# Moving the computation of a branch flag from VectorE to GpSimd, in the first microseconds of a fused attention and MLP kernel

## The reference

```python
scores = scale * np.matmul(q, k.transpose(0, 1, 3, 2))
is_sink = pos[None, :] < int(n_sink)
rel = pos[:, None] - pos[None, :]
in_window = (rel >= 0) & (rel < int(window))
scores = np.where(is_sink | in_window, scores, -1e9)
a = softmax(scores); x = np.matmul(a, v)          # -> 1536 tokens of 512
h = x @ w_in; g = h * tanh(softplus(h)); x = g @ w_out          # first network, 2048 wide
for e in range(4):                                              # second, 4 experts of 1024
    out += p[:, e:e+1] * (relu(x @ w1[e]) @ w2[e])              # p: normalised domain_probs
```

## Time and profile before

| | us |
|---|---|
| median of 3 runs | 852.88 |
| lowest and highest of the runs | 852.72, 852.91 |
| the profiled execution | 852.87 |
| its span in the trace | 851.0 |
| TensorE busy in the span | 842.8 |
| VectorE, ScalarE, GpSimd busy | 605.4, 401.6, 172.1 |

### The profile page before, as it was taken

The page is one execution under the profiler, slowest core; times in us unless marked ns, Lnnn a source line. Parts: engine busy times, 40 slices in busy tenths (PEclk is TensorE's granted clock), DMA queues, the critical chain, the costliest instruction groups (busy, mean ns, idle before and its releaser), DMA issues.

```text
span 851.0 us, 13888 instructions
## 1 busy us (share of the span) xinstructions
PE 842.8 (99%) x4518; PEld 729.6 (86%) x4518; DVE 605.4 (71%) x1170; ACT 401.6 (47%) x739; POOL 172.1 (20%) x259
## 2 busy tenths in 40 slices
PE   7999999999999999999999999999999999999998
PEld 5777888888888888898999899889989998999897
DVE  7888799898888989876566565565565555656655
ACT  6999754448754549754324314314414413422410
POOL 6778200001100112222012112102202202202100
PEclk9999999999999999999999999999999999999999
DMA  7555730004830006825045135225225315403304
GB/s 257 143 162 154 159 100 1 1 0 97 194 106 0 0 0 127 162 59 115 19 104 117 28 89 117 43 74 117 56 61 117 68 49 117 92 25 68 69 0 151
DMA packets 25622, 72.70 MB, mean 85 GB/s; under 512 B 4336, under 2 KB 6512, under 8 KB 25584
## 3 DMA queue, kind: packets, MB, share of 16 engines
q0 software_dynamic: 10720, 33.82, 22.1%
q1 hardware_dynamic: 14576, 38.04, 13.1%
q10 hardware_dynamic: 288, 0.39, 0.1%
HBM read 35.28 MB, written 3.15 MB: 45 GB/s over the span
## 4 chain that ended last, share of the span: by engine, by line
PE 99%; DMA 0%; POOL 0%; DVE 0%; ACT 0%; issue 0%; SPq 0%; DVEq 0%
PE banks L944 31%; PE banks L870 28%; PE banks L839 15%; PE banks L636 15%; PE banks L651 3%; PE banks L732 3%; PE banks L702 3%; PE banks L738 1%; DMA pool<-kT 0%; POOL pool L480 0%; PE banks L705 0%; PE banks L957 0%; ACT pool L1067 0%; DVE pool L1863 0%; DVE pool L1486 0%
## 5 line engine op out<-in xcount | busy, mean ns | idle before, releaser
L1789 DVE SCALAR_TENSOR_TENSOR pool<-banks,p_norm,pool 128x512 f32<-128x512 f32 x179 | 132.8, 748 | 66.1 <-PE banks L944 64.3
L944 PE MATMUL banks<-w_hi,g_lo 128*128 128x512 f32 x382 | 149.9, 392 | 0.0
L944 PE MATMUL banks<-w_lo,g_hi 128*128 128x512 f32 x382 | 149.7, 392 | 0.0
L944 PE MATMUL banks<-w_hi,g_hi 128*128 128x512 f32 x382 | 148.7, 389 | 0.0
L1291 ACT ACTIVATE g_hi<-pool 128x384 fp32r<-128x384 f32 x96 | 50.5, 526 | 190.7 <-DVE pool L1769 139.1
L870 PE MATMUL banks<-x_hi,w_lo 128*128 128x384 f32 x256 | 86.0, 336 | 0.0
L870 PE MATMUL banks<-x_hi,w_hi 128*128 128x384 f32 x256 | 85.9, 335 | 0.0
L870 PE MATMUL banks<-x_lo,w_hi 128*128 128x384 f32 x256 | 85.7, 335 | 0.0
L944 PEld LDWEIGHTS banks<-w_hi,g_lo 128*128 128x128 f32 x382 | 71.7, 188 | 15.0
L944 PEld LDWEIGHTS banks<-w_hi,g_hi 128*128 128x128 f32 x382 | 71.7, 188 | 13.8 <-issue 0.2
L944 PEld LDWEIGHTS banks<-w_lo,g_hi 128*128 128x128 f32 x382 | 71.7, 188 | 13.8
(11 more groups left out here) (151 smaller groups left out, 1776.3 us busy)
## 6 DMA issues: line engine op xcount, KB each, us to landing
w_raw<-weights SPq DMA_DIRECT2D x48, 512.0 KB, 4.4
w_lo<-w_raw POOLq DMA_DIRECT2D x48, 512.0 KB, 5.5
w_lo<-w_sum POOLq DMA_DIRECT2D x15, 384.0 KB, 4.0
pool<-v SPq DMA_DIRECT2D x8, 384.0 KB, 3.5
out<-pool SPq DMA_DIRECT2D x11, 256.0 KB, 2.0
pool<-kT SPq DMA_DIRECT2D x7, 400.0 KB, 5.0
pool<-qT SPq DMA_DIRECT2D x7, 384.0 KB, 4.1
w_lo<-pool POOLq DMA_DIRECT2D x2, 384.0 KB, 4.9
```

What stands on the lines that cost most here:

```text
L944: mm = pe.matmul(banks[:, bank, :], g[:, s, f * SUP + at:f * SUP + at + P], w_cols(w, p2 * SLOT + DOWN_AT[f], DM), start=(f == 0 and n == ...
L1789: dve.scalar_tensor_tensor(out=to, in0=d_bank, scalar=share, in1=to, op0=ALU.mult, op1=ALU.add)\
```

## The change

The five small instructions that make `flag` leave VectorE and are done by GpSimd, behind its identity matrix and ahead of its wide masks, with a new semaphore `ok_made` between the dependent ones. They are written a little differently (one of them does the comparison of the second limit and the product at once). VectorE goes from `lim` straight to its masks. VectorE's read of the flag moves from behind the masking of unit 3 to between unit 1 and unit 2; its branch stays where it was. The other three engines' code is not touched.

```diff
+LIMIT_STEPS = 4
...
+            pl.wait_ge(setup, LIMIT_STEPS)
+            pl.tensor_scalar(ok[:, 0:1], lim[:, 0:1], 0.0, float(SINKS), ALU.max, ALU.min).then_inc(ok_made, 1)
+            pl.tensor_scalar(ok[:, 1:2], lim[:, 1:2], 1.0, float(P), ALU.max, ALU.min).then_inc(ok_made, 1)
+            pl.wait_ge(ok_made, 2)
+            pl.tensor_scalar(ok[:, 2:3], ok[:, 0:1], lim[:, 0:1], None, ALU.is_equal).then_inc(ok_made, 1)
+            pl.wait_ge(ok_made, 3)
+            pl.tensor_scalar(ok[:, 3:4], ok[:, 1:2], lim[:, 1:2], ok[:, 2:3], ALU.is_equal, ALU.mult).then_inc(ok_made, 1)
+            pl.wait_ge(ok_made, 4)
+            pl.tensor_copy(flag[:, :], ok[:, 3:4]).then_inc(flag_ready, 1)
...
-            dve.tensor_scalar(ok[:, 0:1], lim[:, 0:1], 0.0, float(SINKS), ALU.max, ALU.min).then_inc(setup, 1)
-            dve.tensor_scalar(ok[:, 1:2], lim[:, 1:2], 1.0, float(P), ALU.max, ALU.min).then_inc(setup, 1)
+            assert steps[0] == LIMIT_STEPS
             dve.wait_ge(iota_done, 3)
             mask_off(even + P, pos[:, :], sink_limit)
-            dve.wait_ge(setup, steps[0] + 2)
-            dve.tensor_tensor(ok[:, 2:4], ok[:, 0:2], lim[:, :], ALU.is_equal).then_inc(setup, 1)
             mask_off(MASK_AT[0], rel[:, P:], window_limit)
-            dve.wait_ge(setup, steps[0] + 3)
-            dve.tensor_tensor(ok[:, 0:1], ok[:, 2:3], ok[:, 3:4], ALU.mult).then_inc(setup, 1)
             mask_off(MASK_AT[1], rel[:, :], window_limit)
-            steps[0] += 4
-            dve.wait_ge(setup, steps[0])
-            dve.tensor_copy(flag[:, :], ok[:, 0:1]).then_inc(flag_ready, 1)
...
             dve.wait_ge(mask_ready, 5)
-            for u in range(4):
+            for u in range(2):
+                mask_unit(0, u)
+            dve.wait_ge(flag_ready, 1)
+            small = dve.value_load(flag[0:1, 0:1])
+            for u in range(2, 4):
                 mask_unit(0, u)
...
-            dve.wait_ge(flag_ready, 1)
-            small = dve.value_load(flag[0:1, 0:1])
             dve.br_cmp(small, 1, on_true="dve_window", on_false="dve_general", comp_op="IS_EQ")
```

More of the change, by code:

```diff
@@ L300, in build @@
         full_masked = sem("full_masked")
+        ok_made = sem("ok_made")
         qk_in = [sem(f"qk_in{b}") for b in range(B)]
```

## The result

| | us |
|---|---|
| changed kernel, median of 22 runs | 854.03 (853.91 to 854.70) |
| kernel before, median of 22 runs beside it | 852.87 (852.72 to 852.99) |
| ratio | 1.0015, interval 1.0008 to 1.0021 |
| profiled execution, span | 853.91, 852.1 |

The changed kernel is 1.16 us slower. That is inside the 0.2% that the prediction took for what a measurement can tell from no change, and 854.03 lies inside its range of 852.8 to 854.4. But it is nearly twice the 0.65 us of the forecast, it is just outside the "0.3 to 1.1 us slower" to which the prediction gave 0.70, and with 22 runs each the two sets do not overlap. So there is something to explain: half a microsecond.

The account below looks back on a forecast made before the run. The prediction took TensorE, busy 842.8 of 851.0 us, as the bound, movable only through its start at 11.25 us. Flag 0.82 us later less 0.17 slack, +0.65 on 852.87, gave 853.5 us, range 852.8 to 854.4.

Parts of the forecast that it names:

- 0.3 to 1.1 us slower: The forecast case: TensorE's scores of unit 4 wait behind the late flag; chance 0.70.
- When the flag comes now: GpSimd's five instructions (1.27 us) and three gaps of 0.17 us make the flag ready at 6.42 instead of 5.60 us.
- Who waits for the flag: TensorE's scores of unit 4 wait; VectorE's unit 4 starts at 8.76 instead of 8.11 us, 0.65 us later.
- What leaves VectorE: Masks patched some 0.25 us earlier, but VectorE waits for TensorE's scores anyway; gain 0, at most 0.05 us.
- VectorE's read: Ahead of unit 2 its delay is covered; with a flag by 6.3 us it would give back all it gains.
- Rival 2: Flag in time, read hidden in idle time ahead of unit 2; gain at most 0.5 us, 852.4 us; chance 0.05.
- Rival 1: GpSimd's small instructions overlap, flag ready by 5.77 us, TensorE's path within the old slack; 852.9 us; chance 0.12.
- Rival 3: Gap in TensorE's early work delays its full clock; up to 2.5 us more, 856.1 us; chance 0.08.
- TensorE's busy time about the same: Sign of being right: span 0.65 us longer while TensorE's busy time, 842.8 us before, hardly changes.
- The sum: Flag 0.82 us later less 0.17 us of slack: +0.65 us on 852.87, giving 853.5 us.
- Whatever shifts 11.25 shifts the end by the same amount: Premise: TensorE stops waiting at 11.25 us and has no idle time behind; the predicted shift was to 11.90.
- a difference in the span that the shift of TensorE's start does not show: Sign of being wrong, last of those listed: the span changes by something other than TensorE's later start.

Follow-up runs that it names:

- experiment 7: Changed kernel with four spare VectorE memsets restoring its program's place, and GpSimd making the flag in three instructions, window-limit test left out; 852.61 us against 852.78.
- experiment 8: Changed kernel with VectorE's program put back in place, and two more dependent GpSimd instructions ahead of the copy to the flag; 854.07 us.
- experiment 1: Changed kernel with four spare VectorE memsets at its start, putting later VectorE instructions back at their old program places; 853.47 us against 852.85.
- experiment 6: Changed kernel with VectorE's program put back in place by four spare memsets, and VectorE's read of the flag back behind unit 3; 853.55 us.
- experiment 5: Kernel before with only VectorE's read of the flag moved ahead of unit 2, the flag still made on VectorE; 852.71 us against 852.85.
- experiment 3: Kernel before with four instructions taken out of VectorE's attention version that is not run; 853.53 us against 852.85.

## Why the prediction was right, and where it was short

- *When the flag comes now*: right, 6.44 us against 6.42, but by errors that cancel, which is luck: the five instructions took 1.48 us instead of 1.27 (close to the 1.5 us that stood beside the forecast), `lim` was ready 0.04 us earlier, and the gaps between the instructions were shorter than 0.17. All four reads follow it.
- *Who waits for the flag*: right. Flag to TensorE's next scores 0.84 us, unit 4 at 8.72 against 8.76, products at 9.91 against 9.95. Experiments 7 and 8 show that the lateness is what costs, from the point at which the slack is used up at about one for one in the medians, and experiment 1 gives the term its price: 0.62 us, forecast 0.65.
- *What leaves VectorE*: right, nothing. It only waits longer for TensorE.
- *VectorE's read*: right for the late flag (experiment 6: no difference, to 0.1 to 0.2 us). For a flag in time the statement was that the read gives back all that it gains; experiment 5 gives unit 2 at 7.10, as stated, and about 0.1 us of gain, so "all" was slightly too much. Rival 2's gain of up to 0.5 us is refuted.
- *Rival 1* (flag in time) needed the flag by 5.77 us; it came at 6.44. *Rival 3* (TensorE's clock): a gap in TensorE's work did appear, 0.68 us, and the fast pace did come later. The traces record the full granted clock (the higher of the two levels, 2.4 GHz) from 10.5 us in the kernel before, from 12.0 in the changed one, from 11.7 in experiment 1 and from 13.9 in experiment 8; ahead of that they have no record of it. In the changed kernel that was just in time: the transposes at 12.06 us take 273 ns again and the scores behind them start 0.64 us later than before, against 0.61 for the first product. So it explains nothing of the missing 0.5 us, but the margin was small, and in the profiled execution of experiment 8 it was gone. The late flag is not its only cause: with the flag in time in experiment 7 the record starts at 11.2 us. The forecast's "TensorE's busy time about the same" came out at 843.1 against 842.8 us.
- *The sum* was short by 0.5 us. The step that failed is its first premise: "Whatever shifts 11.25 shifts the end by the same amount", because from there on the chain "stays on TensorE". The chain does not end with TensorE; behind its last matmul stands the landing of the last output, and that can change by itself. The list of what the change moves had instructions, waits and issued DMAs in it, and even "No DMA is issued by GpSimd or moved in SyncE's order here", but not the transfers that load the engines' own programs. The page has rows for them, the queues of kind "instruction", and by experiments 1 and 3 their moment depends on how many instructions stand ahead. The sign of being wrong that caught it was the last one: "a difference in the span that the shift of TensorE's start does not show". That 854.03 lies in the forecast range all the same is luck: the range went up to 854.4 for a short delay of the clock, not for a late landing.

The Trainium skill, page "Runtime: NRT & Kernel Launch", section "Instruction fetch mechanics", says that a sequencer fetches its next page through a DMA queue of its own while it executes the current one, and that crossing a page costs little and is mostly hidden. No run here shows a sequencer waiting for its program, and TensorE is busy 100.00 of the 100 us from 20 to 120 us while nine such packets fall there. Packets of kind "instruction" stand on two queues in these traces, q8 with 16 of them in the span and q14 with 22, to which the late one belongs. "Mostly hidden" does not hold at the end: there the fetch lies beside a data transfer on which the time hangs, and costs 0.6 to 0.7 us.

## What to carry to other kernels

- A flag on which several engines branch is waited for by all of them. Here each engine that had nothing else to wait for went on 0.6 to 0.8 us after the flag was ready, 0.5 us of it the read. Put the computation on the engine that finishes it first, not on the one that has time; here the five small instructions cost nothing on VectorE, which waited right behind them, and 0.6 us on GpSimd.
- Before an engine is relieved, look whether it waits right behind. Work taken off ahead of a wait becomes idle time.
- Where differences under 1 us are compared, instructions removed from an engine's program, even in a branch that is not run, can move a program fetch onto the last output transfer, as in experiment 3. Check the DMA queues of kind "instruction" near the end, and shift the program by a few spare instructions before a small loss or gain is put down to the change.

## What the hardware showed that was not expected

- GpSimd's smallest instructions with an input, on 128x1, take 0.19 to 0.42 us (0.19 the copy; 0.21 to 0.42 the scalar operations), with 0.07 to 0.11 us between dependent ones; VectorE's on the same tile take 0.15 us.
- A single 8 KB instruction packet, 0.31 to 0.37 us long, came with a last landing 0.7 us (changed kernel) and 0.9 us (experiment 3) later in the profiled executions, and with 0.56 and 0.68 us in the medians. Four of the 1 KB packets behind it took two to three times their usual 0.046 us.
- The place of an engine's program matters to within a few instructions: four places earlier brought the packet to the end, two places earlier did not.
